# Transposed gate weights: rows turned on TensorE in block 0 in place of a transfer of single words

## The chip, the cores and the metric

One core of one Trainium2 chip runs the whole program. The metric is the device time of one execution in microseconds (us), less is better. The kernel before was run three times: 880.24, 881.27 and 882.05 us, median 881.27 us.

## The reference

Three layers on 2304 tokens of width 512, in float32:

```
attn = softmax(q k^T / 8, causal in blocks of 64) v        # 4 x 8 heads, 576 x 64
x    = attn, heads side by side                            # 2304 x 512
h    = x @ w_in;  g = h > 0 ? h : exp(min(h, 0)) - 1       # 512 -> 2048
x2   = g @ w_out                                           # 2048 -> 512
skip   = x2 @ w_skip;  logits = x2 @ w_gate                # w_gate is 512 x 8
out    = x2;  for tokens with skip > 0:
         e = argmax(logits);  gw = softmax(logits)[e]
         out += gw * (relu(x2 @ w1[e]) @ w2[e])            # 8 experts, 512 -> 1024 -> 512
```

The change touches how `w_gate` (16 KB, 512 rows of 8 words) gets into the layout in which VectorE computes the logits.

## The kernel before

The program has three stages, one after another: attention, feed forward, experts. Each engine has a written-out instruction list; semaphores order them. All transfers but the indirect ones are issued by SyncE (SP), in its program order.

**Feed forward.** The 2304 tokens go in `BLOCKS` = 6 blocks of 384 (three tiles of 128, `TB` = 3); in each block the 2048 hidden columns go in `FC` = 16 chunks of 128. `blocks(step)` walks `step(b, f)` on every engine. In a step TensorE (PE) does `ff_hidden(b, f)`: 12 matmuls of 384 columns, and then `ff_output` of the chunk two steps back (`LAG` = 2): 9 matmuls of 512 columns. Each product is three matmuls (`mm3`, L1549 to L1551), since the operands are split into a high and a low half. ScalarE (ACT) computes the exponential (L1390) and the high half of g (L1396), VectorE (DVE) the rest and the low half (L1228, L1231, L1221).

**Block 0** has more to do: `w_out` comes in 16 pieces of 256 KB through a ring of four buffers (`WR` = 4, `wo_raw`; the profile names them `w_raw`). SP issues piece f (L941) once the low half of piece f - 3 is made, so that piece f - 4 has left the buffer. ACT makes the high half (L1451) at the head of its step f, ahead of the exponential of that step, and GpSimd (POOL) the low half (L1044). PE's `ff_output(0, f)` needs both.

**The gates.** In the blocks before the last, the nine dot products of each token (8 logits and the skip score) are computed on DVE (`dots`, L1110), against `all_gates`: the 8 columns of `w_gate`, each as a row of 512 words, in all 128 partitions. To get there SP first transposes `w_gate` from HBM into an HBM tensor `gates_t` of 8 x 512 (L938), at f = 4 of its loop over the pieces of `w_out`. Past that loop it loads `w_gate` and `w_skip` in their own layout into `gates` (L945, L946; used by TensorE for the last two blocks' logits, L1600), waits for `gates_t`, and broadcasts it to 128 partitions (L930), then `w_skip` (L933), and writes the initial routing table (L950). `dots` starts in block 1 at f = 3. The copy of block 0's result out of PSUM (`x2_copy`, L1422, at f = 2 of block 1) waits for the table's initial write.

**Buffers.** `x2t` (also called `y`) is first used in block 1, by `dots`. The PSUM bank `tr_ps` is first used in the last block.

Of the kernel before, what the change touches and what calls it, by code (L numbers as in the profile page):

```python
# [13 lines left out]
ACT = mybir.ActivationFunctionType  # L14
# [7 lines left out]
P = 128  # L22
# [618 lines left out]
def experts(nc, x2_rows, table, meta, w1, w2, out, w1_raw, w1_in):  # L641

    attn_t, wi, x_raw, w_out, w_skip, w_gate, xr_in = (
        ffn[n] for n in ("attn_t", "wi", "x_raw", "w_out", "w_skip", "w_gate", "x_in"))
    N, DM = out.shape
    F = w_out.shape[0]
    E, _, FE = w1.shape
    KC = DM // P
    FC = F // P
# [21 lines left out]


    DOTS = TB * (LAST - 1)
    DOT_AT = lambda s: RANK_AT(0, s) - 4
    COUNT_AT = RANK_AT(LAST, TB - 1) + 1
    GATHER_AT = COUNT_AT + 1
# [5 lines left out]
    with ExitStack() as ctx:  # L682
# [3 lines left out]
        def sem(name):  # L686
            return ctx.enter_context(nc.semaphore(name))
# [13 lines left out]
        gates = sb("gates", [P, KC, E + 2], F32)  # L701
        ident = sb("ident_f", [P, P], F32)
# [3 lines left out]
        w2_sb = [[w[:, i * FCE:(i + 1) * FCE, :] for w in wo] for i in range(2)]  # L706
        w2_raw = [spare[:, 0], spare[:, 1], x_place[:, 0:2 * DM].rearrange("p (k f) -> p k f", f=DM), spare[:, 2]]
        y = x2t[:, :, :].rearrange("p k t -> p (k t)")
        dot_rows = y.bitcast(BF16).rearrange("p (j d) -> p j d", j=2)
        table_sb = ex[:, :, :].rearrange("p b t -> p (b t)")[:, 0:2 * COLS].bitcast(I32)\  # L710
            .rearrange("p (c w) -> p c w", w=2)
# [24 lines left out]
        gates_t = nc.dram_tensor("gates_t", (E, DM), F32, kind="Internal").ap()  # L736
# [39 lines left out]
        tr_ps = ctx.enter_context(nc.psum_tensor("tr_ps", [P, BANK], F32))  # L776
# [5 lines left out]
        dot_done = sem("dot_done")  # L782
        gates_in = sem("gates_in")
        all_gates_in = sem("all_gates_in")
        gates_turned = sem("gates_turned")
        table_init = sem("table_init")
        wo_in = [sem(f"wo_in{i}") for i in range(WR)]
        wo_hi_done, wo_lo_done = sem("wo_hi_done"), sem("wo_lo_done")
# [113 lines left out]
        @block.sync  # L902
        def _(sp):
            def load_x(b, ks=range(KC)):

                for k in ks:
                    wait(sp, x_lo_done, KC * (b - 1) + k + 1)
                    load_x_rows(sp, attn_t, k, b * NB, x_raw, xr_in)

            def store_x2(b):  # L910
                for s in range(TB):
                    t = TB * b + s
                    sp.wait_ge(x2_done, t + 1)
                    rows = slice(t * P, (t + 1) * P)
                    sp.dma_start(out[rows, :], x2[s][:, :]).then_inc(x2_out[s], 16)
                    sp.dma_start(x2_rows[rows, :], x2[s][:, :]).then_inc(x2_out[s], 16)

            def load_next_w1(e, j):
                wait(sp, w1_lo, PIECES * (e - 1) + j + 1)
                load_w1(sp, w1, e, j, w1_raw, w1_in)  # L920

            def load_w2(e, j):
                if not is_zero(e):
                    wait(sp, w2_lo, PIECES * (e - 1) + j + 1)
                sp.dma_start(w2_raw[j], w2[bass.ds(e, 1), j * FE // PIECES:(j + 1) * FE // PIECES]
                             .rearrange("o (k p) f -> p (o k) f", p=P)).then_inc(w2_in[j], 16)

            def broadcast_gates():
                sp.wait_ge(gates_turned, 16)
                sp.dma_start(all_gates.rearrange("p e d -> p (e d)"),  # L930
                             gates_t.rearrange("(o e) d -> o (e d)", o=1).broadcast_to([P, DM * E]))\
                  .then_inc(all_gates_in, 16)
                sp.dma_start(all_skip, w_skip.rearrange("(o d) -> o d", o=1).broadcast_to([P, DM]))\  # L933
                  .then_inc(all_gates_in, 16)

            for f in range(FC):
                if f == WR:
                    sp.dma_start(gates_t, w_gate.rearrange("d e -> e d"), allow_slow_non_contiguous=True)\  # L938
                      .then_inc(gates_turned, 16)
                wait(sp, wo_lo_done, f - WR + 1)  # L940
                sp.dma_start(wo_raw[f % WR], w_out[f * P:(f + 1) * P, :])\  # L941
                  .then_inc(wo_in[f % WR], 16)
                if f == WR - 1:
                    load_x(1)
            sp.dma_start(gates[:, :, 0:E], w_gate.rearrange("(k p) e -> p k e", p=P)).then_inc(gates_in, 16)  # L945
            sp.dma_start(gates[:, :, E], w_skip.rearrange("(k p) -> p k", p=P),  # L946
                         allow_slow_non_contiguous=True).then_inc(gates_in, 16)
            broadcast_gates()
            sp.wait_ge(const_done, 1)
            sp.dma_start(table.rearrange("(p n) c -> p (n c)", p=P), fill).then_inc(table_init, 16)  # L950

            for b in range(BLOCKS):
                if b + 2 < BLOCKS:
                    load_x(b + 2)
                if b == 1:
                    sp.wait_ge(wo_lo_done, FC)
                    for j in (0, 1):
                        load_w2(0, j)
                if b == LAST - 1:
                    sp.wait_ge(x_lo_done, KC * BLOCKS)  # L960
                    load_w2(0, 2)
                    sp.wait_ge(route, (A_STEPS + B_STEPS) * DOTS)
                    for j in range(PIECES):
                        load_w1(sp, w1, 0, j, w1_raw, w1_in)
                    load_w2(0, 3)
                if b == LAST:
                    for j in range(PIECES):
                        load_next_w1(1, j)
                    for j in range(SLOTS):
                        sp.wait_ge(entered[j], 16 * (BLOCKS // 2 - j // TB))  # L970
                    sp.dma_start(early_sb[:, :], table.rearrange("(p c) w -> p c w", p=P)[:, 0, :])\
                      .then_inc(early_in, 16)
                    for j in range(PIECES):
                        load_w2(1, j)
                store_x2(b)
            for j in range(SLOTS):
                sp.wait_ge(entered[j], 16 * (BLOCKS // 2))
            sp.dma_start(table_sb, table.rearrange("(p c) w -> p c w", p=P)).then_inc(table_in, 16)
            with sp.Fori(2, E) as e:
                for j in range(PIECES):  # L980
                    load_next_w1(e, j)
                for j in range(PIECES):
                    load_w2(e, j)
# [401 lines left out]
        def _(act):  # L1385
            def exp(b, f):
                c = chunk(b, f)
                act.wait_ge(h_done, c + 1)
                wait(act, g_lo_done, c - 1)
                act.activation(ex[:, f % 2], h_ps[:, f % 2, 0:NB], ACT.Exp).then_inc(ex_done, 1)  # L1390
# [57 lines left out]
            def step(b, f):  # L1448
                if b == 0:
                    act.wait_ge(wo_in[f % WR], 16 * (f // WR + 1))  # L1450
                    act.activation(wo[0][:, f, :], wo_raw[f % WR], ACT.Copy).then_inc(wo_hi_done, 1)  # L1451
                if f == LAG and b:
                    x2_copy(b - 1)
                exp(b, f)
                p = back(b, f, 1)
                if p:
                    g_hi(*p)
                if f in X_AT and b < LAST:
                    x_hi(b + 1, X_AT.index(f))
                if b == LAST and f >= HALF:  # L1460
                    if f < HALF + PIECES:
                        act.wait_ge(h_done, chunk(LAST, HALF))
                        w1_high(0, 0, f - HALF)
                    else:
                        act.wait_ge(y_done, chunk(LAST, HALF))
                        w2_high(0, 0, f - HALF - PIECES)
                for s in range(TB):
                    if b:
                        if b == LAST and f == TR_AT(b, s) + 1:
                            x2t_copy(b - 1, s)  # L1470
                        if f == RANK_AT(b, s):
                            soften(b - 1, s)
# [73 lines left out]
        def _(pe):  # L1546
# [76 lines left out]
            def step(b, f):  # L1623
                ff_hidden(b, f)
                p = back(b, f, LAG)
                if p:
                    ff_output(*p)
                if b:
                    for s in range(TB):
                        if b == LAST and f == TR_AT(b, s):  # L1630
                            turn(b - 1, s)
                        if b == LAST and f == TR_AT(b, s) + 2:
                            logits(b - 1, s)
                        if f == RANK_AT(b, s):
                            ranks(b - 1, s)
                if b == LAST and f == COUNT_AT:
                    count(EARLY_T, early_count)
# [160 lines left out]
```

## Time and profile before

| | us |
|---|---|
| median of three timed runs | 881.27 (880.24 to 882.05) |
| profiled execution, whole time | 883.1 |
| its span, first to last instruction | 881.4 |
| PE busy in the span | 815.3 (92%) |
| PE weight loads | 673.5 |
| DVE / ACT / POOL busy | 534.3 / 360.3 / 240.7 |
| mean granted TensorE clock | 0.969 |

Engines are PE (TensorE matmuls), PEld (its weight loads), DVE (VectorE), ACT (ScalarE), POOL (GpSimd), SP (SyncE); a q behind a name is its queue. L938 is line 938 of the kernel. A timeline row gives start, duration, engine, line, operation, out<-in, count and, in brackets, the idle time before it and what ended it. Duration of a matmul is from start to its modelled end; matmuls overlap, so the pace is read from the starts. All times of rows are from the start of the span.

### The profile page before, as it was taken

How to read it: one execution, taken by the hardware profiler on the slowest of the kernel's cores; microseconds unless marked ns; L12 is line 12 of the kernel's file. 1: busy time of each engine (PE TensorE's matmuls, PEld its weight loads, DVE VectorE, ACT ScalarE, POOL GpSimd, SP SyncE). 2: the span in 40 equal slices, each digit the busy share in tenths (PEclk: the TensorE clock that was granted, in tenths of full speed). 3: DMA queues.
4: the chain of work that ended last, by engine and by line, in shares of the span. 5: the costliest groups of instructions: out<-in, count | busy, mean ns of one | idle time of the engine just before them, and what ended most of it. 6: DMA issues, size and time to landing. Idle time of an engine off the chain costs nothing.

```text
span 881.4 us, 14997 instructions
## 1 busy us (share of the span) xinstructions
PE 815.3 (92%) x4726; PEld 673.5 (76%) x4727; DVE 534.3 (61%) x1306; ACT 360.3 (41%) x878; POOL 240.7 (27%) x232
## 2 busy tenths in 40 slices
PE   5999999996906999999999999999998999999995
PEld 4677677774705998889889888889986677887884
DVE  4676677765303337856866865873576699465342
ACT  4766676663203332222223223222345377354241
POOL 3656665561204411201201110210011222221221
PEclk9999999999956999999999999999999899999998
DMA  6344444522863421202002101013133399546100
GB/s 146 98 120 112 118 119 118 152 62 68 63 9 87 129 93 67 67 1 86 24 0 82 28 2 72 25 43 150 48 118 113 113 302 340 200 145 198 35 25 8
DMA packets 101593, 83.30 MB, mean 95 GB/s; under 512 B 67556, under 2 KB 79076, under 8 KB 101416
## 3 DMA queue, kind: packets, MB, share of 16 engines
q1 hardware_dynamic: 98488, 77.68, 31.9%
q0 software_dynamic: 3056, 5.00, 1.8%
q8 instruction: 26, 0.43, 0.2%
q14 instruction: 23, 0.19, 0.1%
HBM read 67.55 MB, written 18.27 MB: 97 GB/s over the span
## 4 chain that ended last, share of the span: by engine, by line
PE 65%; DMA 5%; DVE 2%; issue 1%; ACT 1%; DVEq 0%; POOL 0%; POOLq 0%; ACTq 0%
PE out_ps L1549 11%; PE out_ps L1551 10%; PE h_ps L1549 10%; PE out_ps L1550 10%; PE h_ps L1550 10%; PE h_ps L1551 10%; DMA w_raw<-in_moe_w_out_dram 5%; PE out_ps L1678 1%; PE tr_ps L1643 1%; PE lg_ps L1600 1%; DVE xt_lo L1260 0%; DVE ht_lo L1299 0%; PE tr_ps L1589 0%; DVE x2t L1289 0%; ACT wi_hi L1442 0%
## 5 line engine op out<-in xcount | busy, mean ns | idle before, releaser
L1390 ACT ACTIVATE ex<-h_ps 128x384 f32<-128x384 f32 x96 | 47.3, 493 | 275.8 <-PE h_ps L1551 274.6
L1549 PE MATMUL out_ps<-wo_hi,gt 128*128 128x512 f32 x288 | 115.4, 401 | 31.8 <-DVE gt L1221 31.7
L1228 DVE TENSOR_SCALAR ex<-ex 128x384 f32<-128x384 f32 x96 | 36.2, 378 | 175.4 <-ACT ex L1390 174.3
L1549 PE MATMUL h_ps<-xt_hi,wi_hi 128*128 128x384 f32 x384 | 132.8, 346 | 5.2 <-DVE xt_lo L1260 5.2
L1550 PE MATMUL h_ps<-xt_lo,wi_hi 128*128 128x384 f32 x384 | 130.7, 340 | 0.0
L1551 PE MATMUL h_ps<-xt_hi,wi_lo 128*128 128x384 f32 x384 | 130.5, 340 | 0.0
L1551 PE MATMUL out_ps<-wo_hi,gt 128*128 128x512 f32 x288 | 114.6, 398 | 0.0
L1550 PE MATMUL out_ps<-wo_lo,gt 128*128 128x512 f32 x288 | 114.0, 396 | 0.0
L1549 PEld LDWEIGHTS out_ps<-wo_hi,gt 128*128 128x128 f32 x288 | 54.5, 189 | 41.5 <-issue 32.3
L425 ACT ACTIVATE prob<-s_ps,negmax 128x128 f32<-128x128 f32 (+2 forms) x144 | 78.0, 549 | 13.7 <-DVE negmax L305 7.2
L1110 DVE CUSTOM_DVE_ANT_0 x2t<-x,w_raw 128x512 bf16<-128x512 f32 x108 | 82.7, 807 | 0.4
L1549 PEld LDWEIGHTS h_ps<-xt_hi,wi_hi 128*128 128x128 f32 x384 | 72.8, 190 | 9.2 <-DVE xt_lo L1260 5.8
L1550 PEld LDWEIGHTS h_ps<-xt_lo,wi_hi 128*128 128x128 f32 x384 | 73.1, 190 | 3.2
L1551 PEld LDWEIGHTS h_ps<-xt_hi,wi_lo 128*128 128x128 f32 x384 | 73.0, 190 | 0.0
L1016 POOL DMA_INDIRECT route_table<-entry,slot x18 | 21.0, 1165 | 177.2 <-DVE slot L1189 160.9
L302 DVE TENSOR_REDUCE negmax<-s_ps 128x2 f32<-128x256 f32 (+1 forms) x64 | 51.8, 810 | 28.8 <-PE s_ps L505 28.8
L1008 POOL TENSOR_TENSOR xt_lo<-x_raw,xt_hi 128x384 fp32r<-128x384 f32 x20 | 28.1, 1403 | 143.3 <-ACT xt_hi L1404 143.2
L1551 PEld LDWEIGHTS out_ps<-wo_hi,gt 128*128 128x128 f32 x288 | 54.5, 189 | 13.5
L510 PE MATMUL t_ps<-ident,prob 128*128 128x128 f32 (+1 forms) x400 | 61.5, 284 | 2.0 <-DVE pt L327 0.8
L1550 PEld LDWEIGHTS out_ps<-wo_lo,gt 128*128 128x128 f32 x288 | 54.5, 189 | 9.0
L1549 PE MATMUL out_ps<-wo_hi,ht_hi 128*128 128x512 f32 x120 | 51.5, 429 | 4.5 <-DVE ht_lo L1299 4.2
L1231 DVE TENSOR_TENSOR ex<-h_ps,ex 128x384 f32<-128x384 f32 x96 | 53.5, 558 | 3.3
(174 smaller groups left out, 1673.3 us busy)
## 6 DMA issues: line engine op xcount, KB each, us to landing
w_raw<-in_moe_w_dram SPq DMA_DIRECT2D x56, 512.0 KB, 4.8
attn_t<-attn_sb SPq DMA_DIRECT2D x16, 288.0 KB, 2.2
x_raw<-attn_t SPq DMA_DIRECT2D x24, 192.0 KB, 2.6
out_dram<-x SPq DMA_DIRECT2D x18, 256.0 KB, 2.4
x_rows<-x SPq DMA_DIRECT2D x18, 256.0 KB, 2.8
raw_qk<-in_q_dram SPq DMA_DIRECT2D x32, 128.0 KB, 2.5
raw_qk<-in_k_dram SPq DMA_DIRECT2D x32, 128.0 KB, 2.5
v<-in_v_dram SPq DMA_DIRECT2D x32, 128.0 KB, 2.4
```

The lines of the kernel that those rows point to most:

```text
L302: dve.tensor_reduce(negmax[:, 2 * u:2 * u + 2], s_pair(i, u), AX_X, ALU.max, negate=True).then_inc(max_done, 1)
L425: act.activation(dst, src, ACT.Exp, bias=negmax[:, c:c + 1], accum_out=rowsum[i][:, c:c + 1]).then_inc(exp_done, 1)
L510: return pe.transpose(t_ps[0:src.shape[1], bank, at:at + P], src, ident[:, :])
L1008: pool.tensor_tensor(xtk(b % 2, 1, k), x_raw[k][:, :], xtk(b % 2, 0, k).bitcast(F32), ALU.subtract).then_inc(x_lo_done, 1)
L1016: pool.indirect_dma_start(table, bass.IndirectOffsetOnAxis(ap=slot[j][:, 0:1], axis=0), entry[j][:, :], None, bounds_check=E * N - 1, oob_ ...
L1110: ins = dve.tensor_tensor_reduce(dot_rows[:, ((E + 1) * t + e) % 2], x2[s][:, :], all_skip if e == E else all_gates[:, e, :], 1.0, 0.0, AL ...
L1228: dve.tensor_scalar(e, e, 1.0, -1.0, ALU.min, ALU.add).then_inc(em_done, 1)
L1231: dve.tensor_tensor(e, h_ps[:, f % 2, 0:NB], e, ALU.max).then_inc(g_done, 1)
L1390: act.activation(ex[:, f % 2], h_ps[:, f % 2, 0:NB], ACT.Exp).then_inc(ex_done, 1)
L1549: pe.matmul(dst, stat[0], mov[0], start=start, stop=False, skip_group_check=True)
L1550: pe.matmul(dst, stat[0], mov[1], start=False, stop=False, skip_group_check=True)
L1551: return pe.matmul(dst, stat[1], mov[0], start=False, stop=stop, skip_group_check=True)
```

## The change

`w_gate` and `w_skip` in their own layout are loaded at f = 4 of SP's loop over `w_out`, in place of the transposing transfer, and no longer after it. In block 0 at f = `GATES_AT` = 8 PE waits for them and transposes the four 128 x 8 tiles into `tr_ps`; at f = 9 ACT copies the 8 x 512 result into the first 8 partitions of `x2t` (`gate_rows`). After its loop SP waits for that, stores the 8 rows of 2 KB to `gates_t`, waits for the store, and broadcasts as before.

```diff
--- before.py
+++ after.py
@@ -671,6 +671,7 @@
 
 
     DOTS = TB * (LAST - 1)
+    GATES_AT = FC // 2
     DOT_AT = lambda s: RANK_AT(0, s) - 4
     COUNT_AT = RANK_AT(LAST, TB - 1) + 1
     GATHER_AT = COUNT_AT + 1
@@ -706,6 +707,7 @@
         w2_sb = [[w[:, i * FCE:(i + 1) * FCE, :] for w in wo] for i in range(2)]
         w2_raw = [spare[:, 0], spare[:, 1], x_place[:, 0:2 * DM].rearrange("p (k f) -> p k f", f=DM), spare[:, 2]]
         y = x2t[:, :, :].rearrange("p k t -> p (k t)")
+        gate_rows = y[0:E]
         dot_rows = y.bitcast(BF16).rearrange("p (j d) -> p j d", j=2)
         table_sb = ex[:, :, :].rearrange("p b t -> p (b t)")[:, 0:2 * COLS].bitcast(I32)\
             .rearrange("p (c w) -> p c w", w=2)
@@ -782,7 +784,7 @@
         dot_done = sem("dot_done")
         gates_in = sem("gates_in")
         all_gates_in = sem("all_gates_in")
-        gates_turned = sem("gates_turned")
+        gate_cols_turned, gate_rows_done, gates_turned = sem("gate_cols_turned"), sem("gate_rows_done"), sem("gates_turned")
         table_init = sem("table_init")
         wo_in = [sem(f"wo_in{i}") for i in range(WR)]
         wo_hi_done, wo_lo_done = sem("wo_hi_done"), sem("wo_lo_done")
@@ -925,7 +927,14 @@
                 sp.dma_start(w2_raw[j], w2[bass.ds(e, 1), j * FE // PIECES:(j + 1) * FE // PIECES]
                              .rearrange("o (k p) f -> p (o k) f", p=P)).then_inc(w2_in[j], 16)
 
+            def load_gates():
+                sp.dma_start(gates[:, :, 0:E], w_gate.rearrange("(k p) e -> p k e", p=P)).then_inc(gates_in, 16)
+                sp.dma_start(gates[:, :, E], w_skip.rearrange("(k p) -> p k", p=P),
+                             allow_slow_non_contiguous=True).then_inc(gates_in, 16)
+
             def broadcast_gates():
+                sp.wait_ge(gate_rows_done, 1)
+                sp.dma_start(gates_t, gate_rows).then_inc(gates_turned, 16)
                 sp.wait_ge(gates_turned, 16)
                 sp.dma_start(all_gates.rearrange("p e d -> p (e d)"),
                              gates_t.rearrange("(o e) d -> o (e d)", o=1).broadcast_to([P, DM * E]))\
@@ -935,16 +944,12 @@
 
             for f in range(FC):
                 if f == WR:
-                    sp.dma_start(gates_t, w_gate.rearrange("d e -> e d"), allow_slow_non_contiguous=True)\
-                      .then_inc(gates_turned, 16)
+                    load_gates()
                 wait(sp, wo_lo_done, f - WR + 1)
                 sp.dma_start(wo_raw[f % WR], w_out[f * P:(f + 1) * P, :])\
                   .then_inc(wo_in[f % WR], 16)
                 if f == WR - 1:
                     load_x(1)
-            sp.dma_start(gates[:, :, 0:E], w_gate.rearrange("(k p) e -> p k e", p=P)).then_inc(gates_in, 16)
-            sp.dma_start(gates[:, :, E], w_skip.rearrange("(k p) -> p k", p=P),
-                         allow_slow_non_contiguous=True).then_inc(gates_in, 16)
             broadcast_gates()
             sp.wait_ge(const_done, 1)
             sp.dma_start(table.rearrange("(p n) c -> p (n c)", p=P), fill).then_inc(table_init, 16)
@@ -1451,6 +1456,9 @@
                     act.activation(wo[0][:, f, :], wo_raw[f % WR], ACT.Copy).then_inc(wo_hi_done, 1)
                 if f == LAG and b:
                     x2_copy(b - 1)
+                if b == 0 and f == GATES_AT + 1:
+                    act.wait_ge(gate_cols_turned, 1)
+                    act.activation(gate_rows, tr_ps[0:E, :], ACT.Copy).then_inc(gate_rows_done, 1)
                 exp(b, f)
                 p = back(b, f, 1)
                 if p:
@@ -1625,6 +1633,12 @@
                 p = back(b, f, LAG)
                 if p:
                     ff_output(*p)
+                if b == 0 and f == GATES_AT:
+                    pe.wait_ge(const_done, 11)
+                    pe.wait_ge(gates_in, 32)
+                    for k in range(KC):
+                        last = pe.transpose(tr_ps[0:E, k * P:(k + 1) * P], gates[:, k, 0:E], ident[:, :])
+                    last.then_inc(gate_cols_turned, 1)
                 if b:
                     for s in range(TB):
                         if b == LAST and f == TR_AT(b, s):
```

## Rows read from the trace of the kernel before

**Rows 1.** The page, 40 slices of the span, PE, granted clock, DMA, GB/s

```profile
PE   5999999996906999999999999999998999999995
PEclk9999999999956999999999999999999899999998
```

**Rows 2.** Longest wait of PE over the whole span: us in total, times, longest

```profile
PE out_ps L1549 <- DVE gt L1221: 31.7, 1, 31.7
```

**Rows 3.** Chain that ended last, its piece at 223.79 us: start, length, what

```profile
223.79 45.09 DMA w_raw<-in_moe_w_out_dram
```

**Rows 4.** Timeline of SP's queue, and of ACT across the stall

```profile
222.93 0.81 SPq L938 DMA_DIRECT2D gates_t<-in_moe_w_gate_dram  x1
223.79 31.59 SPq L941 DMA_DIRECT2D w_raw<-in_moe_w_out_dram  x1
...
268.90 0.63 ACT L1451 ACTIVATE wo_hi<-w_raw 128x512 fp32r<-128x512 f32 x1 [35.58 <-DMA w_raw<-in_moe_w_out_dram]
```

**Rows 5.** DMA packets, 222 to 270 us

```profile
DMA packets 5241, 1.85 MB, mean 38 GB/s; under 512 B 4232, under 2 KB 4723, under 8 KB 5240
```

**Rows 6.** Timeline of PE, first matmuls of four successive `ff_output`

```profile
236.40 0.40 PE L1549 MATMUL out_ps<-wo_hi,gt 128*128 128x512 f32 x1
272.50 0.77 PE L1549 MATMUL out_ps<-wo_hi,gt 128*128 128x512 f32 x1 [31.72 <-DVE gt L1221]
279.28 0.40 PE L1549 MATMUL out_ps<-wo_hi,gt 128*128 128x512 f32 x1
283.47 0.40 PE L1549 MATMUL out_ps<-wo_hi,gt 128*128 128x512 f32 x1
```

**Rows 7.** Windows: us, busy (count) of PE, PEld, DVE, ACT, POOL, clock, DMA, GB/s

```profile
248.00:252.00 4.00, 0.00 (x0) 0.00 (x0) 0.00 (x0) 0.00 (x0) 0.00 (x0) 0.50 0.48 0
272.50:278.05 5.55, 5.54 (x15) 4.68 (x15) 2.63 (x3) 1.37 (x3) 2.27 (x2) 0.51 0.44 128
300.00:420.00 120.00, 120.00 (x604) 107.72 (x603) 73.73 (x221) 35.06 (x82) 18.91 (x14) 1.00 0.23 75
540.00:660.00 120.00, 120.00 (x626) 107.56 (x625) 77.19 (x255) 37.61 (x84) 14.35 (x13) 1.00 0.20 68
```

**Rows 8.** DMA issues, 290 to 345 us: KB each, median us from issue to landing

```profile
w_raw<-gates_t SPq DMA_DIRECT2D x1, 2048.0 KB, 8.4
w_raw<-in_moe_w_out_dram SPq DMA_DIRECT2D x3, 256.0 KB, 2.6
x_rows<-x SPq DMA_DIRECT2D x3, 256.0 KB, 2.6
route_table<-x SPq DMA_DIRECT2D x1, 144.0 KB, 9.1
gates<-in_moe_w_gate_dram SPq DMA_DIRECT2D x1, 16.0 KB, 2.6
gates<-in_moe_w_skip_dram SPq DMA_DIRECT2D x1, 2.0 KB, 3.2
```

**Rows 9.** Timeline of PE around four transposes at 606 us

```profile
606.60 0.39 PE L1551 MATMUL out_ps<-wo_hi,gt 128*128 128x512 f32 x1
606.83 0.60 PE L1589 MATMUL tr_ps<-ident_f,x 128*128 128x128 f32 x4
607.18 0.42 PE L1549 MATMUL h_ps<-xt_hi,wi_hi 128*128 128x384 f32 x1
607.44 0.34 PE L1550 MATMUL h_ps<-xt_lo,wi_hi 128*128 128x384 f32 x1
```

**Rows 10.** Timeline of SP's queue, ACT and DVE, 296 to 350 us

```profile
302.79 0.43 SPq L950 DMA_DIRECT2D route_table<-x  x1
...
304.69 0.49 ACT L1390 ACTIVATE ex<-h_ps 128x384 f32<-128x384 f32 x1 [2.79 <-PE h_ps L1551]
...
327.77 1.57 ACT L1422 ACTIVATE x<-out_ps 128x512 f32<-128x512 f32 x3 [1.20 <-PE out_ps L1551]
...
335.93 0.68 DVE L1110 CUSTOM_DVE_ANT_0 x2t<-x,w_raw 128x512 bf16<-128x512 f32 x1
```

## The prediction

> **What bounds the kernel now.** I read the page's slices first. PE is at 9 tenths nearly everywhere, except in slices 10 to 13 (220 to 286 us; a slice is 22 us), where one slice is empty and the granted clock falls to 5 and 6 tenths [rows 1]. So the kernel is bound by PE, save for one hole. The waits of PE say the same in one line: a single wait of 31.7 us for DVE's `gt`, in block 0 [rows 2]. DVE is only the messenger: the chain of work that ended last has at that place one DMA of 45.09 us, a piece of `w_out`, issued at 223.79 [rows 3]. Such a piece needs 2.6 us elsewhere [rows 8].
>
> Why this one took 45 us is in SP's queue: the transfer issued just ahead of it is the transposing one, `gates_t` (L938) [rows 4]. It moves 16 KB as single words, 512 x 8 = 4096 of them. Between 222 and 270 us the trace counts 4232 packets under 512 B, and moves 38 GB/s in all [rows 5]. The piece f = 4 of `w_out` stands behind these words in the same DMA queue. ACT meets its wait for it at the head of its step 4, ahead of that step's exponential, and waits 35.58 us [rows 4]; then DVE has no `ex`, PE has no `gt`, and PE stops.
>
> After the hole the clock is still at 0.51, its 1.2 GHz level, for 5.55 us: it had fallen to 0.50 while PE did nothing, and from 300 to 420 and from 540 to 660 us, with PE busy without a break, it is 1.00 [rows 7].
>
> **What the hole costs, all told.** I take PE's starts, which include the slow clock. `ff_output` begins at 279.28 and next at 283.47, a step of 4.19 us. Two steps before 279.28 it began at 236.40 [rows 6]. Without a hole that would have been 8.38 us earlier, and it was 42.88: 34.50 us are lost. Of these 272.50 - (236.40 + 4.19) = 31.91 are the wait and 6.78 - 4.19 = 2.59 the slow clock after it.
>
> **The change, part by part.** I sum against the profiled execution, 883.1 us.
>
> *Removed: the word transfer.* If nothing else stands ahead of the piece f = 4, all 34.50 us go: -34.50. What is late next must be looked at. Past the hole, ACT's idle time before the exponential of a step in block 0 is 2.79 us and ends with PE's `h_ps` [rows 10], not with a transfer, so the ring of `w_out` keeps up at PE's pace of 4.19 us a step, and PE stays bound by its own matmuls, through 540 to 660 us too [rows 7]. Every later load is issued upon progress of the program, not at a set time, so the saved time is not waited for again. Nothing useful ran under cover of the hole but transfers of this ring.
>
> *Moved: `gates` and `w_skip` in their own layout, to f = 4.* They are 512 pieces of 32 B and 512 of 4 B, and are now ahead of the piece f = 4, which also is issued about 0.1 us later than 223.79 (two issues of some 0.43 to 0.5 us in place of one of 0.81). At their old place they landed 2.6 and 3.2 us after issue [rows 8]. In sequence the piece lands at 223.9 + 3.2 + 2.6 = 229.7. ACT wants it at 268.90 - 35.58 = 233.32 [rows 4], so 3.6 us are to spare: 0. The other bound is the word transfer itself. From its issue at 222.93 to the landing of the piece behind it at 223.79 + 45.09 = 268.88 are 45.95 us, or 11.2 ns for each of 4096 words. At that rate 1024 pieces take 11.5 us and `w_out` lands at 223.9 + 11.5 + 2.6 = 238.0. From ACT's start to PE's took 272.50 - 268.90 = 3.60 us, and PE is due at 236.40 + 4.19 = 240.59, so ACT may start at 236.99. The stall would be 1.0 us, and a clock not yet lowered by such a pause. I take 0, because that row times the very same two transfers, and keep 1.0 for the range. The gain side is closed: PE cannot be earlier than its own matmuls.
>
> The Trainium skill, "DMA: Bandwidth & Descriptors", section Specifications, speaks against this part: transfers want at least 512 bytes apiece for full rate, shorter ones are read and modified before the write. By it these 1024 pieces are of the same kind as the words removed, which is the 11.5 us of the rival below. The row above, 2.6 and 3.2 us, disagrees with so high a price for pieces that go to SBUF.
>
> *Added on PE: four transposes at f = 8.* The waits ahead of them cost nothing: `gates` is in by about 227 us and PE gets there at 236.40 + 4 x 4.19 = 253.2. What is queued behind that wait is all of PE. The four 128-column transposes at 606.83 delay the next matmul by 607.18 - 606.83 = 0.35 us, and the one after it starts 0.26 us later instead of 0.18 [rows 9] (0.18 is the pace of a 384-column matmul: a step of 4.19 less nine of 0.23, over twelve). In all +0.43 us, and PE is the bound, so it counts in full. Here only 8 columns are turned, but the moving side is 128 columns of the identity again, so I take the same; bounds 0 and 0.60, the length of the group.
>
> *Added on ACT: the copy of 8 x 512 at f = 9.* Nearest is the copy of 128 x 512 out of PSUM, 1.57 us for three [rows 10]: about 0.5. ACT has 2.79 us idle in each step, spent on `h_ps`, and the result of PE's step 8 is there before PE's `h_ps` of step 9 can be. So 0; without that cover +0.5.
>
> *Added on SP, after its loop: a store of 8 rows and a wait for its landing.* Stores to HBM land after 2.6 us [rows 8]; with the issue 3.0 us, less about 1.1 for the two loads that moved away. Behind that wait stand the broadcast, `w_skip`, the table's initial write and the next block's loads, all about 2 us later in relation to PE. The tightest is the table: issued at 302.79, landed 9.1 us later at 311.9 [rows 8, 10], and ACT's copy that waits for it runs at 327.77: 15.9 us to spare. The broadcast is issued before the table's write and landed by 302.79 + 8.4 = 311.2; `dots` wants it at 335.93 [rows 10]: 24.7 us to spare. If the store took the 9.1 us of the slowest transfer there, 8 us would still fit. So 0.
>
> **Sum.** 883.1 - 34.50 + 0.43 = 849.0. The profiled execution is 1.8 us above the median of the runs, 881.27, so the median should be 847.2.
>
> **Rivals.**
> - *The small pieces delay `w_out` like the words did* (the skill's rule above). They are words again, and in the same queue. Against it is the row of 2.6 and 3.2 us. Price 1.0 us worked out above, and up to 2.6 more for a slow clock if it falls: 848.2 to 850.8. Chance 0.12.
> - *The rows' way to `all_gates` is too long: slower than before.* The place is SP's new wait for the store. If it lasts T, the table's initial write lands T - 1.1 later and ACT stops in block 1 once T is above 15.9 + 1.1 = 17 us; beyond that PE loses each microsecond, and the kernel is slower than before once T is over 17 + 34.1 = 51 us, 881.3 or more. Only the word transfer itself was ever as slow (45.95 us at most), a store of 2 KB rows was 2.6. Chance 0.01; a T of 17 to 51, a part of the gain, 0.02.
> - *The hole was not the words' doing:* the piece f = 4 is late for another reason, for example the four x loads just ahead, and the hole stays. Then 881.3 + 0.4 = 881.7, no change. Against it are the 4232 small packets and the idle rate of 38 GB/s. Chance 0.02.
> - *Only a part goes*, because the w_out ring, refilled during the hole, proves too slow when it has no pause. Each step with a late piece costs a few tenths: some 3 us over ten steps, 850. The 2.79 us of idle time on ACT that end with PE speak against it. Chance 0.08.
>
> **How the numbers follow.** The forecast, 847.2, has 0.75. Its own range is +-1.5 for what runs differ by (880.24 to 882.05 before) and the transposes' bounds. The range is carried up to 851.5 to take in the first and the last rival, and down to 845.0. A difference under 0.2% (1.8 us) can't be told from no change; faster than that are all cases but the second (slower) and the third (same).
>
> **What would show it.** In the profile after: no wait of PE above about 3 us in block 0 and no empty slice in the PE row; `w_out` pieces landing in at most some 6 us; the clock at 1.00 from 224 us on; PE idle 31.7 us less, PE busy about 2 us less for the matmuls that ran at the low clock; `all_gates` and the table landed more than 10 us before their readers. I am wrong if PE waits in block 0 for a `w_out` piece behind the gates' loads, if ACT or DVE waits for the table or the broadcast in block 1, or if PE's idle time turns up again behind block 0.

## The result, and the profile after

The changed kernel takes 851.39 us (median of 4 runs, 849.3 to 853.47) against 880.75 us of the kernel before (median of 4: the three runs given above and 879.74): ratio 0.9666, 95% interval 0.9638 to 0.9693. The forecast was 847.2, range 845.0 to 851.5. The profiled execution took 851.58 us, its span is 849.9 us, PE is busy for 96% of it, mean clock 0.987.

The page's slices, as in [rows 1]: the empty slice is gone, and the clock's two low slices with it. The 7 tenths in slice 11 are the fall between attention and block 0, 216.3 to 226.6 us; before has such a fall too (216.5 to 223.4), split between two slices.

```profile
PE   5999999998799999999999999999997999999995
PEclk9999999999799999999999999999999999999998
```

PE's waits from 210 us on (us in total, times, longest), as in [rows 2]. The 31.7 us are gone. The first three were there before (5.2, 4.2 and 1.5 us); the wait for `x_now` was not, but it comes and goes between runs of either kernel (experiment 7).

```profile
PE h_ps L1557 <- DVE xt_lo L1265: 5.3, 2, 4.8
PE out_ps L1557 <- DVE ht_lo L1304: 4.1, 4, 2.5
PE h_ps L1557 <- DVE m_xt_lo L1299: 1.5, 1, 1.5
PE tr_ps L1657 <- DVE x_now L1285: 1.2, 1, 1.2
```

SP's queue, as in [rows 4] and [rows 10]: where the transfer of single words stood are the two loads. Behind the loop the store of the 8 rows goes at 268.19 and the broadcast at 270.62, 2.4 us later: that is the new wait.

```profile
222.93 0.44 SPq L931 DMA_DIRECT2D gates<-in_moe_w_gate_dram  x1
223.41 0.51 SPq L932 DMA_DIRECT2D gates<-in_moe_w_skip_dram  x1
223.96 44.18 SPq L949 DMA_DIRECT2D w_raw<-in_moe_w_out_dram  x12
268.19 0.38 SPq L937 DMA_DIRECT2D gates_t<-x2t  x1
270.62 0.35 SPq L939 DMA_DIRECT2D w_raw<-gates_t  x1
...
271.49 0.43 SPq L955 DMA_DIRECT2D route_table<-x  x1
```

Landing of the 16 pieces of `w_out`: 2.6 us in the median, the longest 4.4, where it was 45.1.

```profile
DMA to landing us min/median/max: 2.4/2.6/4.4
```

PE and ACT around the turned gates, as in [rows 9]. From the first transpose to the next matmul of `ff_hidden` are 257.14 - 256.79 = 0.35 us. ACT had waited 0.69 us of time in which it had nothing else to do.

```profile
256.79 0.60 PE L1640 MATMUL tr_ps<-ident_f,gates 128*8 128x128 f32 x4
257.14 0.42 PE L1557 MATMUL h_ps<-xt_hi,wi_hi 128*128 128x384 f32 x1
257.40 0.34 PE L1558 MATMUL h_ps<-xt_lo,wi_hi 128*128 128x384 f32 x1
...
257.42 0.59 ACT L1461 ACTIVATE x2t<-tr_ps 8x512 f32<-8x512 f32 x1 [0.69 <-PE tr_ps L1640]
```

The deadlines in block 1, as in [rows 10]: the table (issued 271.49, landed 8.9 us later, 280.4) is read at 295.22, with 14.8 us to spare; the broadcast landed at 277.9 and `dots` starts at 303.38.

```profile
295.22 1.58 ACT L1427 ACTIVATE x<-out_ps 128x512 f32<-128x512 f32 x3 [1.20 <-PE out_ps L1559]
...
303.38 0.68 DVE L1115 CUSTOM_DVE_ANT_0 x2t<-x,w_raw 128x512 bf16<-128x512 f32 x1
```

**How runs differ.** I cut each profile at the last matmul of attention, at the first copy of block 0's result, at the last such copy of the last block, and at the end of the last scatter (us):

| profile | attention ends | to block 0's result | to the last block's | to the last scatter |
|---|---|---|---|---|
| before, first | 214.2 | 113.6 | 340.8 | 207.0 |
| before, e11 | 215.0 | 111.7 | 340.8 | 208.9 |
| before, e12 | 214.4 | 111.1 | 340.8 | 208.8 |
| changed, first | 214.0 | 81.2 | 340.8 | 208.0 |
| changed, e8 | 214.5 | 79.8 | 340.8 | 206.9 |

### The profile page after: what moved, and what is told of

It is laid out like the page before. It is cut to its first block, busy times and chain, and to the rows that moved or that the text cites. A ratio compares the mean times of both kernels' runs of the same rounds, so it can differ in the third digit from the quotient of the medians.

```text
span 849.9 us, 15007 instructions
## 1 busy us (share of the span) xinstructions
PE 814.4 (96%) x4730; PEld 673.6 (79%) x4731; DVE 532.2 (63%) x1306; ACT 360.8 (42%) x879; POOL 240.9 (28%) x232
## 4 chain that ended last, share of the span: by engine, by line
PE 69%; DVE 2%; issue 1%; DVEq 1%; ACT 0%; POOL 0%; POOLq 0%; ACTq 0%
PE h_ps L1557 11%; PE out_ps L1557 11%; PE h_ps L1558 11%; PE h_ps L1559 11%; PE out_ps L1559 11%; PE out_ps L1558 11%; PE out_ps L1692 1%; PE tr_ps L1657 1%; PE lg_ps L1608 1%; DVEq L858 0%; DVE xt_lo L1265 0%; PE tr_ps L1597 0%; DVE ht_lo L1304 0%; DVE x2t L1294 0%; DVE tile_ids L1274 0%
## 5 line engine op out<-in xcount | busy, mean ns | idle before, releaser
L425 ACT ACTIVATE prob<-s_ps,negmax 128x128 f32<-128x128 f32 (+2 forms) x144 | 78.0, 549 | 13.7 <-DVE negmax L305 7.2
L265 POOL TENSOR_TENSOR qk_hi<-qk_f,one 128x512 fp32r<-128x512 f32 (+1 forms) x30 | 36.0, 1200 | 71.1 <-ACT qk_f L406 61.1
```

Source lines behind the costliest of these rows:

```text
L265: pool.tensor_tensor(qk_hi[i][:, a:b], qk_f[i][:, a:b], one[:, :].to_broadcast([P, b - a]), ALU.mult).then_inc(split_hi, 1)
L425: act.activation(dst, src, ACT.Exp, bias=negmax[:, c:c + 1], accum_out=rowsum[i][:, c:c + 1]).then_inc(exp_done, 1)
```

## The experiments

Nine kernels, and the changed one and the one before profiled again. They ran in three jobs; each ratio is to the kernel before in the same job, whose median was 881.18 us (experiments 1 to 4), 881.14 (5 to 7) and 880.73 (8 to 10).

**1. The words put back.** Into the changed kernel, after `load_gates()`:

```diff
+                    sp.dma_start(unused[:, 0:512], w_gate[0:512, :].rearrange("d e -> e d"),
+                                 allow_slow_non_contiguous=True).then_inc(unused_in, 16)
```

> The changed kernel with the transfer of 4096 single words put back ahead of the piece f = 4 of w_out, into a tensor that nobody reads. Theory A (the words block the queue for 45 us, everything else of the change is free): PE again has one wait of some 32 to 37 us in block 0, the clock falls to 0.50, the median is 882 to 888 us. Rival B (it was the order of the loads, not the words): about 851, as the changed kernel, with no wait in block 0.

884.87 us, ratio to before 1.0035 (1.0016 to 1.0054). The hole is back, 2 us short of the expected 32. The last gap ahead of `ff_output`, PE's timeline, and the landing of the transfers into `w_raw`, of which the piece behind the words is the longest:

```profile
271.53 0.77 PE L1562 MATMUL out_ps<-wo_hi,gt 128*128 128x512 f32 x1 [29.85 <-DVE gt L1231]
...
DMA to landing us min/median/max: 2.4/2.8/41.9
```

So the gain is the absence of this one transfer. That is shown, not argued. What is not explained: the median is 3.7 us above the 881.18 of before, and the interval excludes 1. The profile, at 882.66 us the third fastest of ten runs, has nothing of it: block 0's result comes 111.0 us after attention's end, against 111.1 to 113.6 before (the table above). So something of the change may cost up to 3.7 us while the words are there; without them no such cost is seen (in one job 851.13 us for the kernel before with the words walked the other way, experiment 8, and 850.77 for the changed one, experiment 9).

**2. Half the words** (`unused[:, 0:256]`, `w_gate[0:256, :]`).

> As the kernel with the words put back, but with 2048 of the 4096. Theory A, cost per word 11.2 ns and a slack of 3.6 us ahead of ACT plus 3.7 behind it: the wait of PE is 23 us shorter, 9 to 14 us, median 861 to 867 us. Rival C (a fixed cost of the transfer, not one per word): the wait stays above 25 us, median over 876.

870.34 us, ratio 0.9891 (0.9869 to 0.9912).

```profile
256.40 0.77 PE L1562 MATMUL out_ps<-wo_hi,gt 128*128 128x512 f32 x1 [13.63 <-DVE gt L1231]
...
DMA to landing us min/median/max: 2.5/3.1/27.7
```

The wait is inside what was expected, the median 3.3 us above. Half the words took 16.2 us off the wait of experiment 1 and not the 23 that 11.2 ns a word give. The cost grows with the words, but not from zero: the piece f = 4 lands 27.7 us after issue with 2048 words ahead of it and 41.9 with 4096 (experiment 1), so the second half costs (41.9 - 27.7) / 2048 = 6.9 ns a word and the first half more: (27.7 - 3.0) / 2048 = 12.1 ns, against the 3.0 us of the piece without words. My 11.2 ns is an average, and no price for another count.

**3. The words from ACT's queue.** In the kernel before, L938 is taken from SP, and ACT issues it at its step 1:

```diff
+                    if f == 1:
+                        act.dma_start(gates_t, w_gate.rearrange("d e -> e d"), allow_slow_non_contiguous=True)\
+                           .then_inc(gates_turned, 16)
```

> The kernel before, with its transfer of 4096 words issued from ACT's queue at step 1 of block 0 in place of SP's queue at f = 4; nothing else. Theory Q (the pieces of w_out wait behind the words in the same queue): from another queue the words pass beside them, w_out lands in under 8 us, no long wait of PE, median 849 to 853. Rival E (the words fill the DMA engines themselves, whoever issues them): the pieces of w_out take over 20 us again, PE waits 15 us or more, median over 865.

875.81 us, ratio 0.9942 (0.9913 to 0.9972): theory Q, which is how I had put it in the prediction ("in the same queue"), falls, and rival E comes out. The ten runs spread from 872.66 to 881.13 us, and the profiled one, 879.72, is among the longer ones; theory Q's 849 to 853 is far from all of them. ACT's timeline has the words in one queue and a `w_out` piece of the other stuck all the same; this is piece f = 5, issued at 228.19, which took 40.3 us to land. Piece f = 4 was issued at 224.31, just ahead of the words, and landed after 3.3 us.

```profile
224.80 1.31 ACTq L1448 DMA_DIRECT2D gates_t<-in_moe_w_gate_dram  x1
...
268.51 0.63 ACT L1451 ACTIVATE wo_hi<-w_raw 128x512 fp32r<-128x512 f32 x1 [28.29 <-DMA w_raw<-in_moe_w_out_dram]
...
DMA to landing us min/median/max: 2.6/3.7/40.3
```

So the words hold up transfers of the other queue too; whether it is in the DMA engines or at HBM, this run can't tell. The Trainium skill says that transfers of all issuing engines run on the same 16 DMA engines ("DMA: Bandwidth & Descriptors", Issuing engines are not separate DMA queues), and the 40.3 us agree with that.

**4. The words moved behind the loop, alone.** In the kernel before the transfer stands first in `broadcast_gates()` and not at f = 4.

> The kernel before, with its transfer of 4096 words moved behind the loop over w_out, and nothing else. The hole in block 0 goes (-34.5 us), but SP now waits some 35 to 45 us for the words before it issues the broadcast and the table's initial write, and ACT's copy in block 1 has 15.9 us to spare: a new wait of PE of some 15 to 27 us in block 1, with up to 2.6 us of slow clock behind it. Theory A: median 866 to 879. Rival (all words are as good as hidden once w_out is not behind them): about 848 to 851.

878.67 us, ratio 0.9991 (0.9969 to 1.0013), at the upper end of theory A. The hole moves to block 1: ACT's copy waits for the table, 25.3 us, and PE for the copy. SP issued the words at 269.79 and the broadcast at 309.72.

```profile
269.79 0.81 SPq L929 DMA_DIRECT2D gates_t<-in_moe_w_gate_dram  x1
309.72 0.35 SPq L932 DMA_DIRECT2D w_raw<-gates_t  x1
...
PE out_ps L1548 <- ACT x L1421: 23.8, 1, 23.8
...
319.92 1.57 ACT L1421 ACTIVATE x<-out_ps 128x512 f32<-128x512 f32 x3 [25.33 <-DMA route_table<-x]
```

This bears out the deadline read from [rows 10]: with some 40 us in place of the store's 2.4, the 15.9 us to spare are used up. Moving the transfer gained nothing that the interval can tell from 0; it had to become short.

**5. The transposes ten times over** (`for k in [k for _ in range(10) for k in range(KC)]`).

> The changed kernel with its four transposes issued ten times over, 36 more. By the pace of the row of before (0.35 us for four) PE's block 0 is 3.2 us longer, the median 3 to 4 us above the changed kernel beside it. By a price of 0.275 us each, which the Trainium skill gives for a transpose (TensorE: Matmul & The Clock Gate, Part 4: PE-mode transpose), 9.9 us. If they lower the clock as well, more than 10.

854.99 us, ratio to before 0.9704 (0.9690 to 0.9718), beside 850.57 of the changed kernel in the same job (experiment 6): 4.4 us more, 0.4 above what was expected. In the trace the 40 transposes delay the next matmul by 262.51 - 258.22 = 4.29 us, 0.107 each, 3.94 more than the four. The granted clock stays at 1.00 through them and behind them. So the change's transposes cost 0.43 us as taken (0.35, and 257.40 - 257.14 = 0.26 for the next matmul in place of 0.18), and the Trainium skill's 0.275 us apiece are not their pace: one lasts 0.273 us in the trace, but they overlap.

```profile
258.22 4.53 PE L1640 MATMUL tr_ps<-ident_f,gates 128*8 128x128 f32 x40
262.51 0.42 PE L1557 MATMUL h_ps<-xt_hi,wi_hi 128*128 128x384 f32 x1
```

**6. The changed kernel once more.**

> The changed kernel once more, for the phase of the clock: by the first profiles the granted clock rose to full 3.2 us later in block 0 than before (1.6 us lost) and fell once more in the expert stage (1.5 us lost). If that is chance of the run and not of the change, this profile shows the rises and falls at other times: block 0 ends 31 to 34.5 us earlier than in the first profile of before, the median is 849 to 853. If it belongs to the change, they stand at the same places within 0.3 us, and the median is 850.5 to 852.

850.57 us (849.5 to 851.8), ratio 0.9665 (0.9651 to 0.9679). The clock rose in block 0 at other points: in the first profile of the changed kernel it is at 0.50 up to 226.6 us, here up to 224.2, in the three of before up to 223.4, 225.5 and 223.9. It is the run, not the change. Windows of one microsecond of the first profile of before, of the first of the changed kernel, and of this one (columns as in [rows 7]):

```profile
223.00:224.00 1.00, 1.00 (x6) 1.00 (x6) 0.00 (x0) 0.23 (x1) 0.00 (x0) 0.82 0.90 297
```

```profile
223.00:224.00 1.00, 1.00 (x4) 1.00 (x4) 0.00 (x0) 0.05 (x1) 0.00 (x0) 0.50 0.99 355
225.00:226.00 1.00, 1.00 (x5) 1.00 (x5) 0.43 (x1) 0.00 (x0) 0.96 (x1) 0.50 0.93 180
```

```profile
224.00:225.00 1.00, 1.00 (x7) 1.00 (x7) 0.18 (x1) 0.70 (x2) 0.00 (x0) 0.90 0.92 202
```

**7. PE's idle time filled.** To the changed kernel, at the end of attention and ahead of block 0:

```diff
             all_steps(step)(pe)
+            for _ in range(14):
+                pe.matmul(s_ps[:, 0:BANK], qk_hi[0][:, 0:P], qk_hi[0][:, 0:BANK], start=True, stop=True)
...
+            for _ in range(6):
+                pe.matmul(lg_ps[:, :], wi[0][:, 0, 0:P], wi[0][:, 0, 0:BANK], start=True, stop=True)
             blocks(step)
```

> The changed kernel with matmuls that nobody reads in PE's idle time between attention and feed forward: 14 at the end of attention and 6 ahead of block 0, some 4.6 us in a hole of 4.8. If the slow clock at the head of block 0 is due to that idle time, the granted clock stays 1.00 from 216 to 227 us, and the 0 to 1.6 us go that the slow matmuls behind DVE's last low half cost: median 0.5 to 1.6 us under the changed kernel. Rival: idle time is not what lowers it, the clock falls to 0.50 there all the same and the time is the same or up to 1 us longer.

And with three fillers more in the expert stage, `fill(tr_ps, 10)` ahead of `output(0, 0, ...)`, `fill(tr_ps, 5)` ahead of `turn_x(1)`, `fill(lg_ps, 6)` behind the wait for `route`:

> As the kernel with the filled start, with 21 more matmuls that nobody reads in three pauses of PE at the head of the expert stage (2.5, 1.2 and 1.5 us). If idle time is what lowers the clock, it stays 1.00 through both, and 3 to 5 us go against the changed kernel: median 846 to 849. Rival: the fillers delay real work by 0.5 to 2 us and nothing is gained, 850 to 853.

851.04 and 850.08 us, ratios to before 0.9667 (0.9654 to 0.9680) and 0.9656 (0.9641 to 0.9671). Windows of the unfilled kernel (experiment 6) and of the second filled one, ahead of block 0 and in the expert stage:

```profile
219.00:220.00 1.00, 0.73 (x2) 0.73 (x3) 0.97 (x4) 0.00 (x0) 0.85 (x4) 0.50 0.92 287
650.00:651.00 1.00, 1.00 (x4) 0.76 (x3) 0.53 (x4) 0.11 (x1) 0.00 (x0) 0.50 0.02 8
```

```profile
219.00:220.00 1.00, 1.00 (x5) 0.82 (x6) 0.96 (x5) 0.00 (x0) 0.99 (x9) 1.00 0.26 18
650.00:651.00 1.00, 1.00 (x5) 0.77 (x5) 0.18 (x2) 0.74 (x1) 0.00 (x0) 1.00 0.08 25
```

With the idle time filled the clock stays at 1.00 in the filled places, and in no others: the first filled kernel still has 0.50 in the expert stage. Every profile without the fillers has 0.50 in both. So idle time is what lowers it. The gain that I expected is not there: neither differs from the changed kernel by more than the intervals. From attention's end to block 0's result are 79.7 us in the second, which the plain kernel reached in e8 too (79.8). In the expert stage it takes 206.9 us, as e8 with its 6.8 us of low clock: with the filler PE waits for DVE instead (1.6 us for `x_now`).

The expert stage of all 14 profiles shows why so little hangs on it. In 13 the clock is low for 6.8 us in all, and the stage has three lengths, by where these lie (us; the first column counts from the last block's last copy):

| clock at 0.50 | PE's wait for `x_now` | to the last scatter | profiles |
|---|---|---|---|
| 12 to 19 | none | 206.9 to 207.0 | before first, e8, experiment 4 |
| 13 to 18 and 23 to 28 | 1.2 | 207.8 to 208.1 | changed first, experiments 1, 3, 5, 7 (start filled), 8 |
| 22 to 29 | 2.7 | 208.8 to 208.9 | e11, e12, experiments 2 and 9 |
| nowhere | 1.6 | 206.9 | experiment 7 (all filled) |

The early low clock costs nothing against no low clock at all; where it comes late the stage is up to 2 us longer. That the early one is free because PE would wait for `x_now` in that time is my reading of the second column, and not tested.

**8. The same words in another order.** In the kernel before, one line:

```diff
-                    sp.dma_start(gates_t, w_gate.rearrange("d e -> e d"), allow_slow_non_contiguous=True)\
+                    sp.dma_start(gates_t.rearrange("e d -> d e"), w_gate, allow_slow_non_contiguous=True)\
```

> The kernel before, with the same 4096 words from HBM to HBM at the same place, but walked as 512 rows of 8 (reads in order, writes as single words apart) and not as 8 rows of 512. Theory S (a transfer is shared out among the 16 DMA engines by its outermost count: 8 rows reach 8 of them; the Trainium skill, DMA: Bandwidth & Descriptors, How many engines (k)): twice the engines, the words take about half as long, 18 to 26 us, PE's wait falls to 8 to 15 us, median 860 to 868. Rival W (the number of words or their writes in HBM set the time, whoever moves them): PE's wait stays at 28 to 34 us, median 878 to 884.

851.13 us, ratio 0.9654 (0.9615 to 0.9692). Both theories fall short: it is not twice as fast but three times. The piece behind the words lands after 13.7 us (42.9 in e12), and ACT waits 4.29 us, PE 0.5. So this one line alone, with nothing turned on TensorE, brings the time of the changed kernel.

```profile
w_raw<-in_moe_w_out_dram SPq DMA_DIRECT2D x1, 256.0 KB, 13.7
gates_t<-in_moe_w_gate_dram SPq DMA_DIRECT2D x1, 16.0 KB, 13.7
...
238.29 0.63 ACT L1451 ACTIVATE wo_hi<-w_raw 128x512 fp32r<-128x512 f32 x1 [4.29 <-DMA w_raw<-in_moe_w_out_dram]
```

**9. As many words, to SBUF.** To the changed kernel, after `load_gates()`:

```diff
+                    for k in range(KC):
+                        sp.dma_start(unused[:, :, k], w_gate[k * P:(k + 1) * P, :],
+                                     allow_slow_non_contiguous=True).then_inc(unused_in, 16)
```

> The changed kernel with 4096 single words in front of the piece f = 4 of w_out again, in four transfers of 1024, but written to SBUF (128 partitions x 32 words, nobody reads them) and not to HBM. Theory N (the number of pieces is what costs): 10 ns a word as before, the piece takes some 40 us, PE waits 28 to 34 us, median 880 to 886. Theory H (words to HBM are dear, words to SBUF are not; 1024 small pieces to SBUF landed in 3 us): under 12 us for all of them, PE waits 0 to 6 us, median 850 to 857.

850.77 us, ratio 0.9654 (0.9613 to 0.9694). Theory H, as to SBUF: each transfer of 1024 words lands in 2.7 to 3.3 us, and `w_out` pieces in at most 4.3. The first line is of the words' transfers, the second of `w_out`'s.

```profile
DMA to landing us min/median/max: 2.7/2.7/3.3
...
DMA to landing us min/median/max: 2.3/2.8/4.3
```

**10. The kernel before, two more profiles.**

> The kernel before, for one more profile. The first profile stood 2.2 us above the median of its runs. If that excess lay in the hole, it is shorter here than 31.7 us, and the changed kernel gains less against a usual run of before than against the first profile. If it lay elsewhere (attention, the clock in the expert stage), the hole is 31.7 us within 0.3.

> The kernel before, a third profile, for the same question: hole of 29 to 31 us, or 31.7 again.

883.84 and 882.52 us, and the hole is 29.2 and 29.4 us, not 31.7. (The first profile, 883.1, stands 1.8 us above 881.27, the median of its runs, not 2.2.) PE's longest wait in each:

```profile
PE out_ps L1549 <- DVE gt L1221: 29.2, 1, 29.2
```

```profile
PE out_ps L1549 <- DVE gt L1221: 29.4, 1, 29.4
```

Both executions were long for other reasons than the hole: their expert stage took 1.9 and 1.8 us more than the first one's (the table above).

## Why the prediction was right, and where it was off

**The hole, its cause and its price** held. PE's wait of 31.7 us and the slow clock behind it are gone, nothing took their place, and putting the words back brings the hole back and the old time, but for 3.7 us that stay unexplained (experiment 1). One reading of the slices was off, without effect: the empty slice and the one behind it are the 12th and 13th, 242 to 286 us; the 10th is short because of PE's pause ahead of block 0. What was off in the cause is the queue: I had the words block `w_out` because both were in SP's queue. They block it from another queue as well (experiment 3).

**The moved loads** cost nothing: they landed, and the piece behind them took 3.0 us. What I had drawn from the Trainium skill's rule of 512 bytes ("DMA: Bandwidth & Descriptors", Specifications), that these small pieces are as dear as the words, did not hold here; the rule itself, which is about full rate, no run here tests. Experiment 9 goes further: 4096 words to SBUF are not dear either. What was dear was this walk of 8 rows of 512 words from HBM to HBM (experiment 8).

**The transposes** at 0.43 us and **ACT's copy** at 0 were as taken. **SP's wait for the store** was 2.4 us in place of 3.0, the table had 14.8 us to spare. Experiment 4 is the rival of the long way to `all_gates` made true: some 40 us in that place, between the 17 and 51 of that rival, took back nearly all of the gain. By that rival's sum it should have been 40 - 17 = 23 us; the profile is 28.1 us above that of experiment 6 (877.58 and 849.5). The wait itself is 23.8; behind it the clock is at 0.50 for 5.4 us more, of which about half is lost; the last 1.6 us I can't place.

**The sum** is 4.2 us too low (847.2 against 851.39), and the terms that were missing are these. In the profiled execution I forecast 849.0 and it took 851.58, 2.6 more. Block 0's result came 327.77 - 295.22 = 32.55 us earlier where -34.50 + 0.43 says 34.07: 1.5 us, the clock that rose 3 us later at the head of block 0. The last 1.0 us is the table's last column, 208.0 against 207.0: the low clock of the expert stage is as long in both, but half of it lies later in the changed kernel's (experiment 7). Both are chance of the run (experiment 6). The remaining 1.6 us is the step "1.8 us above the median of the runs ... so the median should be 847.2". It took the first profile's excess for something that both kernels share. It was not: a good part of it was in the hole itself, 31.7 us there and 29.2 and 29.4 in two other runs (experiment 10), and it went with the hole; the changed kernel's profile is just 0.2 above its median. How long the hole was in the timed runs, which have no trace, is not shown. The mean of my three profiles of before and two of after gives 112.1 - 80.5 = 31.6 us for block 0, the medians of two jobs 29.4 and 30.6 us for the whole; I can't close that last microsecond with five profiles.

**The range held by luck.** The forecast's own range, 847.2 with +-1.5 us, does not reach 851.39. The range was carried up to 851.5 for two rivals, `w_out` delayed by the gates' loads and a ring that is too slow, and neither came. What filled that room is something else: the subtraction above and the places of the low clock, which the prediction took as the same before and after. Two of its signs failed for the same reason: the clock was not at 1.00 from 224 us on (0.50 up to 226.6 us, and twice in the expert stage), and PE was busy for 0.9 us less (815.3 to 814.4), not 2.

**The rivals.** The hole that stays, and the part that is eaten by a slow ring of `w_out`, did not come: the pieces land in 4.4 us at most.

## What to carry to other kernels

Where an engine waits long for a load, look at what was issued just before it, on any queue, count its packets by size, and see where they go: a 16 KB transfer from HBM to HBM held up a 256 KB one for 40 us here, and as many single words to SBUF held up nothing. If such a transfer must stay, try its walk the other way round first: one line here, 8 x 512 to 512 x 8, gave the same time as turning the tiles on TensorE, storing and waiting. And when one removes a hole, the profile's excess over the median may be the hole's own: price it from several profiles before carrying it over.

## What the runs showed of the hardware beyond that

- 4096 single words from HBM to HBM, with one 256 KB piece behind them: 41.9 to 45.1 us to the piece's landing walked as 8 rows of 512, 13.7 us walked as 512 rows of 8; four transfers of 1024 words to SBUF, 3.3 us at most each. By the Trainium skill's rule ("DMA: Bandwidth & Descriptors", Why a DMA increments its semaphore by 16 and not by 1, How many engines (k)) the first walk runs on 8 DMA engines and the second on 16, which as an estimate gives a factor of two. How many engines took part no view here shows. Whether the rest is due to the order of reads, of writes, or to the landing in HBM is open: I did not try a walk that changes one alone.
- Between attention and block 0 PE did nothing for 4.8 us, and in that time or just behind it the granted clock fell to 0.50 (1.2 GHz); with 20 matmuls that nobody reads in that place it stayed at 1.00 (2.4 GHz). The time was the same within the intervals.
- In the expert stage the same 6.8 us at 0.50 cost between 0 and 2 us, by where they lay (experiment 7).
- Executions of one kernel differ by up to 2.5 us from attention's end to block 0's result and by up to 1.9 us in the expert stage, while the five blocks between take 340.8 us in all five profiles of the two kernels.
